# Attention and two MLPs on one core: one transfer per head for q and k, loads reordered, all sum units added on GpSimd

## The chip, the cores and the metric

The kernel runs on one core of a Trainium2 chip. The metric is the device time of one execution in microseconds (us). Five engines work side by side and meet at semaphores: TensorE (PE), VectorE (DVE), ScalarE (ACT), GpSimd (POOL) and SyncE (SP), which here does nothing but issue transfers. Transfers are carried by 16 DMA engines that all queues share.

## The reference

Inputs are q, k and v of 2 batches x 12 heads x 448 rows x 64 in float32, a number `cap` (30), and the weights of two MLPs of 768 and 2048 columns.

```python
scores = np.matmul(q, k.transpose(0, 1, 3, 2)) / np.sqrt(64)
scores = cap * np.tanh(scores / cap)
scores = scores - np.max(scores, axis=-1, keepdims=True)
attn = np.exp(scores)
attn = attn / (np.sum(attn, axis=-1, keepdims=True) + 1e-09)
x = np.matmul(attn, v)            # then heads side by side: 896 x 768
x = relu(x @ w_in1) ** 2 @ w_out1
x = silu(x @ w_in2) @ w_out2
```

## The kernel before

**Work.** The 24 heads are 12 pairs. One "slot" of PE handles one pair: scores of pair j (three pieces of 128 key rows for both heads, one of 64), and, between them, the product of the weights with v of pair j-1 and the sum of its weights. After slot 11 the two MLPs follow, which are matrix products alone: weights are split in a high and a low part (ACT writes `w_hi`, DVE writes `w_lo`), and each product is three matmuls (lines 371 to 373).

**Loading.** A head's rows are dealt to partitions so that partition i holds rows 14i to 14i+13, 896 numbers that lie together in memory. DVE transposes blocks of 32 x 32 (lines 582 and 586 into `qk_f`), and a head dimension of 64 needs two groups of 32 partitions: the first half of every row's 64 columns in one, the second half in the other. The kernel loads the same 32 x 896 numbers twice, into the two groups, the first group shifted by 32 columns, so that one strided view of `qk_raw` reads the first half of the columns in one group and the second in the other. That makes four transfers for k of a pair and four for q (line 190). v takes four transfers of 32 partitions for `v_t` (line 200) and four for `v_x` (line 206). A pair thus takes 16 transfers.

**Order on SP.** k of pair 0, q and k of pair 1, v of pairs 0 and 1, the first two weight tiles (line 212), q and k of pair 2. Then `load_pair(j)` in a loop: wait until pair j-1 is transposed (`s_turned`), load q and k of pair j+1; wait until the sums of pair j-2 are done (`s_att`), load v of pair j. There are two `qk_raw` buffers. q of pair 0 is issued by ACT (line 455).

**Weights and sums.** ACT takes tanh of the scores (lines 464, 467) and the exponential in two pieces (line 472, 1792 and 1344 columns). A pair's weights are 7 units of 448 columns: units 0 to 3 in the first piece, 4 to 6 in the second. POOL adds units 0,1 and 2,3 (line 275) and then, once for each head, the half unit 6 (line 280). PE sums down the partitions with matmuls against ones (`sums`, line 333): two read POOL's sums and two read units 4 and 5 as they are. They leave four groups of 32 partitions, and DVE joins them (`finish`: line 603 copies four pieces into `den_x`, line 605 adds), takes the reciprocal and scales the output.

**What stands late.** ACT's `weight_high` (line 495) for weight tile 0 stands after pair 1, the one for tile 1 between pair 10 and pair 11. PE's first MLP work starts with line 371 after slot 11.

Of the kernel before, what the change touches and what calls it, by code (L numbers as in the profile page):

```python
# [13 lines left out]
P = 128  # L14
DMA = 16


def attention_then_two_mlps(nc, q, k, v, cap, w_in1, w_out1, w_in2, w_out2, out):
# [28 lines left out]

    q_v = q.rearrange("b (m h) (i t) d -> (b m) h i (t d)", h=2, t=QB)
    k_v = k.rearrange("b (m h) (i t) d -> (b m) h i (t d)", h=2, t=QB)
    v_v = v.rearrange("b (m h) (i t) d -> (b m) i h (t d)", h=2, t=QB)  # L50
    w_in_v = [w.rearrange("(k p) f -> p k f", p=P) for w in (w_in1, w_in2)]
# [4 lines left out]
    with ctx:  # L56
# [14 lines left out]
        eps_t = sb(ctx, "eps_t", [P, 1])  # L71
        o_sel = sb(ctx, "o_sel", [P, BL])
        w_raw = [sb(ctx, f"w_raw{i}", [P, WK, P]) for i in range(2)]
# [5 lines left out]
        with ExitStack() as att:  # L79

            qk_raw = [sb(att, f"qk_raw{i}", [P, BL + 2 * QB * D]) for i in range(2)]
# [12 lines left out]
            rowmax = sb(att, "rowmax", [P, 2, S])  # L94
            den_r = sb(att, "den_r", [P, S])
            den_x = sb(att, "den_x", [P, QB])
# [86 lines left out]
        def _(sp):  # L183
            def load_part(j, n, src, done):

                for h in range(2):
                    for a in range(2):
                        at = n * QB * D + BL * (1 - a)
                        rp = slice(D * h + BL * a, D * h + BL * a + BL)
                        sp.dma_start(qk_raw[j.par][rp, at:at + QB * D],  # L190
                                     src[bass.ds(j.no, 1), h][0]).then_inc(done, DMA)

            def load_qk(j):
                load_part(j, 0, k_v, s_qk_in[j.par])
                load_part(j, 1, q_v, s_qk_in[j.par])

            def load_v(j):
                for g in range(C):
                    at = g * CW * D
                    sp.dma_start(v_t[j.par][BL * g:BL * g + BL, :, :],  # L200
                                 v_v[bass.ds(j.no, 1), :, :, at:at + CW * D][0]).then_inc(s_v_in[j.par], DMA)
                for h in range(2):
                    for g in range(XB):
                        at = (MB + g) * D
                        rp = slice(D * h + BL * g, D * h + BL * g + BL)
                        sp.dma_start(v_x[j.par][rp, :],  # L206
                                     v_v[bass.ds(j.no, 1), :, h, at:at + D][0]).then_inc(s_v_in[j.par], DMA)

# [11 lines left out]

            load_part(At(0, 0), 0, k_v, s_first_in[0])
            sp.wait_ge(s_first_in[0], 4 * DMA)
            load_qk(At(0, 1))
            for j in range(2):
                load_v(At(0, j))
            for f in range(2):
                load_w_in(0, At(0, f), At(0, f))
            sp.wait_ge(s_turned, 2)
            load_qk(At(0, 2))

            def load_pair(j):
# [34 lines left out]
        def _(pool):  # L266
# [3 lines left out]
            def add_units(j):  # L270

                wait(pool, s_att, j.no - 1)
                pool.wait_ge(s_exp, 2 * j.no + 1)
                t, a = prob[j.par], asum[j.par]
                pool.tensor_tensor(a[:, :, :], t[:, 0:2, :], t[:, 2:4, :], ALU.add).then_inc(s_sum, 1)
                pool.wait_ge(s_exp, 2 * j.no + 2)
                for h in range(2):
                    rp = slice(D * h, D * h + D)
                    pool.wait_ge(s_sum, 3 * j.no + 1 + h)
                    pool.tensor_tensor(a[rp, h, :], a[rp, h, :], t[rp, 2 * CW, :], ALU.add).then_inc(s_sum, 1)  # L280
                pool.wait_ge(s_sum, 3 * j.no + 3)

# [16 lines left out]
        def _(pe):  # L299
# [27 lines left out]
            def sums(j):  # L327

                pe.wait_ge(s_sum, 3 * j.no + 3)
                for g in range(4):  # L330
                    h = g // 2
                    mov = asum[j.par][:, h, :] if g % 2 == 0 else prob[j.par][:, 4 + h, :]
                    last = pe.matmul(o_t[j.par][BL * g:BL * g + BL, 1, 0:S], o_sel[:, :], mov,  # L333
                                     start=True, stop=True)
                last.then_inc(s_att, 1)

            def output_main(j):
                pe.wait_ge(s_v_in[j.par], 8 * DMA * (j.half + 1))
# [111 lines left out]
        def _(act):  # L450
            for h in range(2):
                for a in range(2):
                    at = QB * D + BL * (1 - a)
                    rp = slice(D * h + BL * a, D * h + BL * a + BL)
                    act.dma_start(qk_raw[0][rp, at:at + QB * D], q_v[0, h]).then_inc(s_first_in[1], DMA)
            off_max = shifted(act)
# [107 lines left out]
        def _(dve):  # L564
            dve.memset(o_sel[:, :], 1.0).then_inc(s_fill, 1)
            dve.memset(eps_t[:, :], EPS).then_inc(s_eps_t, 1)
# [9 lines left out]
            def blocks(j, first, last):  # L576

                return qk_raw[j.par][:, BL + first * D:BL + last * D].rearrange("p (t x) -> p t x", x=D)[:, :, 0:BL]

# [9 lines left out]
            def prepare(j):  # L589
                dve.wait_ge(s_qk_in[j.par], 8 * DMA * (j.half + j.par))  # L590
                wait(dve, s_score, C * (j.no - 1))
# [3 lines left out]
            def finish(j):  # L595

                dve.wait_ge(s_att, j.no + 1)
                dve.transpose(den_r[:, :], o_t[j.par][:, 1, 0:S]).then_inc(s_den, 1)
                dve.wait_ge(s_den, 8 * j.no + 1)
                part = den_r[:, :].rearrange("p (b i) -> p b i", i=BL)[:, :, 0]  # L600
                for g in range(4):
                    o = g + 1 - 2 * (g % 2)
                    dve.tensor_copy(den_x[BL * g:BL * g + BL, :], part[BL * o:BL * o + BL, :]).then_inc(s_den, 1)
                dve.wait_ge(s_den, 8 * j.no + 5)
                dve.scalar_tensor_tensor(den[:, :], part, eps_t[:, 0:1], den_x[:, :],
                                         op0=ALU.add, op1=ALU.add).then_inc(s_den, 1)
                dve.wait_ge(s_den, 8 * j.no + 6)
                dve.reciprocal(den[:, :], den[:, :]).then_inc(s_den, 1)
                dve.wait_ge(s_den, 8 * j.no + 7)
                dve.transpose(rinv[:, :].rearrange("p (b i) -> p b i", i=BL),  # L610
                              den[:, :].unsqueeze(2).to_broadcast([P, QB, BL])).then_inc(s_den, 1)
                dve.wait_ge(s_den, 8 * j.no + 8)
                dve.tensor_tensor(att_o[:, :], o_t[j.par][:, 0, 0:S], rinv[:, :], ALU.mult).then_inc(s_norm, 1)  # L613
# [158 lines left out]
```

## Time and profile before

| | us |
|---|---|
| median of 3 runs | 587.06 (586.62 to 587.24) |
| profiled execution | 586.58 |
| its span in the profile | 584.8 |
| PE busy | 565.7 (97%) |
| DVE / ACT / POOL busy | 223.1 / 167.4 / 54.3 |

The span runs from the first to the last recorded instruction, and 1.8 us of the profiled time lie outside it. In the rows of the timeline a number in front is the start in us, the next the time from the first start to the last end of the merged instructions, and brackets give the idle time just before and what ended it. "SPq" rows are SP's issuing of transfers, not the transfers themselves.

### The profile page before, as it was taken

What the parts mean: (1) busy time and instruction counts of PE and PEld (TensorE: products, weight loads), DVE (VectorE), ACT (ScalarE), POOL (GpSimd) and SP (SyncE); (2) the same over time, 40 slices, a digit from 0 to 9 for tenths busy, and PEclk for the clock granted to TensorE, in tenths of its full rate; (3) what the DMA queues carried; (4) which work ended last, traced back from release to release, by engine and by line L of the source; (5) the groups of instructions that cost most, each with busy time, mean ns of one, the idle gap of its engine ahead of it and who ended that gap; (6) DMA issues with size and microseconds to landing.
All of it is one profiled execution on the core that took longest, in us unless ns stands there. A gap on an engine that the chain in (4) does not pass through costs nothing.

```text
span 584.8 us, 7972 instructions
## 1 busy us (share of the span) xinstructions
PE 565.7 (97%) x2800; PEld 466.0 (80%) x2800; DVE 223.1 (38%) x403; ACT 167.4 (29%) x207; POOL 54.3 (9%) x42
## 2 busy tenths in 40 slices
PE   5599999999999999999999999999999999999996
PEld 3133333499999999999999999999999999999996
DVE  2177977975555555121202123333333302120210
ACT  4578888422222222021202113222222201010100
POOL 1535655400000000000000000000000000000000
PEclk9989999999999999999999999999999999999999
DMA  5745544211111122212121102111112221212553
GB/s 141 188 106 155 146 129 123 67 34 56 54 54 54 55 62 67 69 39 69 41 66 40 49 28 67 56 53 55 54 54 62 62 66 47 62 46 63 92 86 48
DMA packets 83122, 41.93 MB, mean 72 GB/s; under 512 B 27808, under 2 KB 80032, under 8 KB 83104
## 3 DMA queue, kind: packets, MB, share of 16 engines
q1 hardware_dynamic: 81952, 41.13, 26.4%
q10 hardware_dynamic: 1120, 0.57, 0.5%
q8 instruction: 10, 0.16, 0.1%
q14 instruction: 8, 0.07, 0.0%
q0 software_dynamic: 32, 0.00, 0.0%
HBM read 38.93 MB, written 2.75 MB: 71 GB/s over the span
## 4 chain that ended last, share of the span: by engine, by line
PE 90%; SPq 4%; DMA 2%; DVE 2%; issue 1%; DVEq 0%
PE ring L371 13%; PE o_t L371 13%; PE o_t L373 13%; PE ring L373 13%; PE ring L372 13%; PE o_t L372 13%; PE o_t L324 4%; PE ring L312 3%; SPq L190 2%; DMA qk_raw<-in_q_dram 1%; PE o_t L333 1%; PE ring L309 1%; PE o_t L322 1%; SPq L206 1%; DMA qk_raw<-in_k_dram 1%
## 5 line engine op out<-in xcount | busy, mean ns | idle before, releaser
L689 DVE TENSOR_TENSOR w_lo<-w_raw,w_hi 128x768 fp32r<-128x768 f32 (+1 forms) x56 | 60.0, 1072 | 292.6 <-ACT w_hi L495 292.6
L495 ACT ACTIVATE w_hi<-w_raw 128x768 fp32r<-128x768 f32 (+1 forms) x56 | 52.5, 938 | 358.8 <-PE ring L373 182.8
L371 PE MATMUL ring<-x_hi,w_hi 128*128 128x448 f32 x384 | 140.4, 366 | 0.0
L371 PE MATMUL o_t<-g_hi,w_hi 128*128 128x448 f32 x384 | 140.2, 365 | 0.0
L373 PE MATMUL o_t<-g_hi,w_lo 128*128 128x448 f32 x384 | 140.2, 365 | 0.0
L372 PE MATMUL ring<-x_lo,w_hi 128*128 128x448 f32 x384 | 140.2, 365 | 0.0
L372 PE MATMUL o_t<-g_lo,w_hi 128*128 128x448 f32 x384 | 140.2, 365 | 0.0
L373 PE MATMUL ring<-x_hi,w_lo 128*128 128x448 f32 x384 | 140.2, 365 | 0.0
L371 PEld LDWEIGHTS ring<-x_hi,w_hi 128*128 128x128 f32 x384 | 72.1, 188 | 7.2 <-issue 1.5
L372 PEld LDWEIGHTS o_t<-g_lo,w_hi 128*128 128x128 f32 x384 | 72.1, 188 | 5.7
L371 PEld LDWEIGHTS o_t<-g_hi,w_hi 128*128 128x128 f32 x384 | 72.1, 188 | 5.7
L373 PEld LDWEIGHTS o_t<-g_hi,w_lo 128*128 128x128 f32 x384 | 72.1, 188 | 5.7
L373 PEld LDWEIGHTS ring<-x_hi,w_lo 128*128 128x128 f32 x384 | 72.1, 188 | 5.7
L372 PEld LDWEIGHTS ring<-x_lo,w_hi 128*128 128x128 f32 x384 | 72.1, 188 | 5.7
L312 PE MATMUL ring<-qk_f 64*128 64x448 f32 x144 | 35.2, 594 | 11.3 <-DVE qk_f L586 9.1
L467 ACT ACTIVATE prob<-ring,qk_scale 128x896 f32<-128x896 f32 x36 | 35.0, 1002 | 19.5 <-PE ring L312 19.5
L312 PEld LDWEIGHTS ring<-qk_f 64*128 64x128 f32 x144 | 12.6, 193 | 32.9 <-issue 28.4
L472 ACT ACTIVATE prob<-prob,cap_a 128x1792 f32<-128x1792 f32 (+1 forms) x24 | 38.5, 1602 | 0.8
L663 DVE TENSOR_TENSOR g_lo<-work,g_hi 128x448 f32 (+1 forms) x64 | 36.9, 618 | 0.0
L324 PE MATMUL o_t<-prob,v_t 128*64 128x448 f32 x144 | 30.7, 562 | 0.9 <-DVE att_o L613 0.6
L513 ACT ACTIVATE work<-ring 128x448 f32<-128x448 f32 x64 | 30.7, 531 | 0.0
L280 POOL TENSOR_TENSOR asum<-asum,prob 64x448 f32<-64x448 f32 x24 | 28.2, 1177 | 18.3 <-ACT prob L472 17.3
(44 smaller groups left out, 249.9 us busy)
## 6 DMA issues: line engine op xcount, KB each, us to landing
w_raw<-in_moe_w_in_dram SPq DMA_DIRECT2D x32, 384.0 KB, 3.4
w_raw<-in_moe_w_out_dram SPq DMA_DIRECT2D x24, 512.0 KB, 3.9
qk_raw<-in_k_dram SPq DMA_DIRECT2D x48, 112.0 KB, 2.4
qk_raw<-in_q_dram SPq DMA_DIRECT2D x44, 112.0 KB, 2.5
out_dram<-rows SPq DMA_DIRECT2D x46, 56.0 KB, 2.2
v_t<-in_v_dram SPq DMA_DIRECT2D x48, 48.0 KB, 1.8
v_x<-in_v_dram SPq DMA_DIRECT2D x48, 8.0 KB, 1.6
qk_raw<-in_q_dram ACTq DMA_DIRECT2D x4, 112.0 KB, 4.3
```

The costliest lines, as they stand in the source:

```text
L280: pool.tensor_tensor(a[rp, h, :], a[rp, h, :], t[rp, 2 * CW, :], ALU.add).then_inc(s_sum, 1)
L312: last = pe.matmul(ring[2 * (u % 2) + h][:, 0:S], qk_f[j.par][rp, u * P:u * P + P], qk_f[j.par][rp, S:2 * S], start=True, stop=True)
L324: pe.matmul(out_h, v_t[j.par][:, h, c * D:c * D + D], prob[j.par][:, 2 * c + h, :], start=(c == 0), stop=False)
L371: pe.matmul(dst, w_hi[par][:, kk, :], mov_hi, start=start, stop=False)
L372: pe.matmul(dst, w_hi[par][:, kk, :], mov_lo, start=False, stop=False)
L373: return pe.matmul(dst, w_lo[par][:, kk, :], mov_hi, start=False, stop=stop)
L467: act.activation(prob[j.par][:, 2 * u:2 * u + 2, :], ring2[u % 2][:, :, 0:S], ACT.Tanh, scale=qk_scale[:, 0:1]).then_inc(s_ring, 1)
L472: act.activation(t, t, ACT.Exp, scale=cap_a[:, 0:1]).then_inc(s_exp, 1)
L495: act.activation(w_hi[n.par][:, 0:blocks, :], w_raw[n.par][:, 0:blocks, :], ACT.Copy).then_inc(s_w_hi, 1)
L513: act.activation(work[f.par][b][:, :], ring[2 * f.par + b][:, 0:S], ACT.Relu if layer == 0 else ACT.Silu).then_inc(s_ring, 1)
L663: dve.tensor_tensor(g_lo[:, bass.ds(f.no, 1), b, :], work[f.par][b][:, :].unsqueeze(1), g_hi[:, bass.ds(f.no, 1), b, :].bitcast(F32), ALU. ...
L689: dve.tensor_tensor(w_lo[n.par][:, 0:blocks, :], w_raw[n.par][:, 0:blocks, :], w_hi[n.par][:, 0:blocks, :].bitcast(F32), ALU.subtract).the ...
```

## The change

1. **q and k.** One transfer per head fills both groups of 32 partitions. Its source pattern starts with a dimension of count 2 (the two column halves, 32 numbers apart), then 32 rows, then 864 numbers; the destination is 64 partitions x 864. A pair takes four such transfers instead of eight. The bytes are nearly the same (864 instead of 896 numbers a partition), and a transfer carries twice as many.
2. **v.** `v_t` takes one transfer per head: source counts 4, 32, 192, destination 128 partitions. `v_x` takes one per head: source counts 2, 32, 64, destination 64 partitions. A pair takes four instead of eight.
3. **SP's order.** v of pair 1 is issued after q and k of pair 2, and the first two weight tiles after `load_pair(10)` instead of before pair 2. ACT's and DVE's steps for these tiles move with them.
4. **Sums.** POOL adds units 4,5 too, in one more 128 x 896 addition. PE then needs two matmuls of 64 columns for a pair's sums instead of four of 32, and DVE one addition (`eps`) instead of four copies and an addition.

```diff
+    def halves(t):
+        flat = t.rearrange("b (m h) (i t) d -> (b m) h (i t d)", h=2, t=QB)
+        def head(n, h):
+            first = flat[n, h] if isinstance(n, int) else flat[bass.ds(n, 1), h][0]
+            return bass.AP(first.tensor, first.offset, [[BL, 2], [QB * D, BL], [1, QB * D - BL]])
+        return head
+    q_v, k_v = halves(q), halves(k)
+    v_flat = v.rearrange("b (m h) (i t) d -> (b m) h i (t d)", h=2, t=QB)
+    v_main = v_flat[:, :, :, 0:MB * D].rearrange("n h i (g x) -> n h g i x", g=C)
+    v_rest = v_flat[:, :, :, MB * D:QB * D].rearrange("n h i (g x) -> n h g i x", g=XB)
...
             def load_qk(j):
-                load_part(j, 0, k_v, s_qk_in[j.par])
-                load_part(j, 1, q_v, s_qk_in[j.par])
+                for n, src in enumerate((k_v, q_v)):
+                    for h in range(2):
+                        sp.dma_start(qk_raw[j.par][D * h:D * h + D, n * QB * D:(n + 1) * QB * D - BL],
+                                     src(j.no, h)).then_inc(s_qk_in[j.par], DMA)
...
             def load_v(j):
+                for h in range(2):
+                    rp = slice(D * h, D * h + D)
+                    sp.dma_start(v_t[j.par][:, h, :], v_main[bass.ds(j.no, 1), h][0]).then_inc(s_v_in[j.par], DMA)
+                    sp.dma_start(v_x[j.par][rp, :], v_rest[bass.ds(j.no, 1), h][0]).then_inc(s_v_in[j.par], DMA)
...
             load_qk(At(0, 1))
-            for j in range(2):
-                load_v(At(0, j))
-            for f in range(2):
-                load_w_in(0, At(0, f), At(0, f))
+            load_v(At(0, 0))
             sp.wait_ge(s_turned, 2)
             load_qk(At(0, 2))
+            load_v(At(0, 1))
...
             load_pair(At(0, PAIRS - 2))
+            for f in range(2):
+                load_w_in(0, At(0, f), At(0, f))
...
                 pool.wait_ge(s_exp, 2 * j.no + 2)
+                pool.wait_ge(s_sum, 4 * j.no + 1)
+                pool.tensor_tensor(a[:, :, :], a[:, :, :], t[:, 4:6, :], ALU.add).then_inc(s_sum, 1)
...
-                for g in range(4):
-                    h = g // 2
-                    mov = asum[j.par][:, h, :] if g % 2 == 0 else prob[j.par][:, 4 + h, :]
-                    last = pe.matmul(o_t[j.par][BL * g:BL * g + BL, 1, 0:S], o_sel[:, :], mov,
+                for h in range(2):
+                    last = pe.matmul(o_t[j.par][D * h:D * h + D, 1, 0:S], ones[:, :], asum[j.par][:, h, :],
                                      start=True, stop=True)
...
-            weight_high(At(0, 0), KC)
             two_steps(act, 2, PAIRS - 4, weights)
             weights(At(0, PAIRS - 2))
-            weight_high(At(0, 1), KC)
+            for f in range(2):
+                weight_high(At(0, f), KC)
             weights(At(0, PAIRS - 1))
```

SP's queue from its start to the loads of pair 2, before (the shapes are those of the destination; x4 means four in a row; `s_first_in` is the arrival of k of pair 0, `s_turned` the transposes of pair 0):

```order
L190 DMA qk_raw<-in_k_dram 32x896 x4
L190 DMA qk_raw<-in_k_dram 32x896 [waits s_first_in0]
L190 DMA qk_raw<-in_k_dram 32x896 x3
L190 DMA qk_raw<-in_q_dram 32x896 x4
L200 DMA v_t<-in_v_dram 32x2x192 x4
L206 DMA v_x<-in_v_dram 32x64 x4
L200 DMA v_t<-in_v_dram 32x2x192 x4
L206 DMA v_x<-in_v_dram 32x64 x4
L212 DMA w_raw<-in_moe_w_in_dram 128x6x128 x2
L190 DMA qk_raw<-in_k_dram 32x896 [waits s_turned]
L190 DMA qk_raw<-in_k_dram 32x896 x3
L190 DMA qk_raw<-in_q_dram 32x896 x4
```

The same place now:

```order
L218 DMA qk_raw<-in_k_dram 64x1x864 x2
L196 DMA qk_raw<-in_k_dram 64x1x864 [waits s_first_in0]
L196 DMA qk_raw<-in_k_dram 64x1x864
L196 DMA qk_raw<-in_q_dram 64x1x864 x2
L202 DMA v_t<-in_v_dram 128x1x192
L203 DMA v_x<-in_v_dram 64x1x64
L202 DMA v_t<-in_v_dram 128x1x192
L203 DMA v_x<-in_v_dram 64x1x64
L196 DMA qk_raw<-in_k_dram 64x1x864 [waits s_turned]
L196 DMA qk_raw<-in_k_dram 64x1x864
L196 DMA qk_raw<-in_q_dram 64x1x864 x2
```

Between the arrival of k of pair 0 and the first load of pair 2 stood 26 transfers, and now there are 8.

ACT's queue from the end of pair 10 to the start of pair 11, before (`s_w_in1` is the arrival of weight tile 1, `s_score` a finished piece of scores):

```order
L472 ACTIVATE prob<-prob,cap_a 128x1344 [waits s_ring]
L484 UNCONDITIONAL_BRANCH
L495 ACTIVATE w_hi<-w_raw 128x768 [waits s_w_in1]
L467 ACTIVATE prob<-ring,qk_scale 128x896 [waits s_att,s_score]
L467 ACTIVATE prob<-ring,qk_scale 128x896 [waits s_score]
```

The same place now:

```order
L466 ACTIVATE prob<-prob,cap_a 128x1344 [waits s_ring]
L478 UNCONDITIONAL_BRANCH
L489 ACTIVATE w_hi<-w_raw 128x768 [waits s_w_in0]
L489 ACTIVATE w_hi<-w_raw 128x768 [waits s_w_in1]
L461 ACTIVATE prob<-ring,qk_scale 128x896 [waits s_att,s_score]
L461 ACTIVATE prob<-ring,qk_scale 128x896 [waits s_score]
```

The step for tile 0 stood after pair 1 and is now here too, so both wait ahead of pair 11's first tanh.

## Rows read from the trace of the kernel before

**Rows 1.** The page, busy shares and 40 slices of 14.6 us

```profile
PE 565.7 (97%) x2800; PEld 466.0 (80%) x2800; DVE 223.1 (38%) x403; ACT 167.4 (29%) x207; POOL 54.3 (9%) x42
...
PE   5599999999999999999999999999999999999996
...
PEclk9989999999999999999999999999999999999999
DMA  5745544211111122212121102111112221212553
```

**Rows 2.** Timeline of PE: starts of slots 1, 2, 3, 4, 5, 11, then the MLP

```profile
14.31 1.77 PE L312 MATMUL ring<-qk_f 64*128 64x448 f32 x8 [0.88 <-ACT prob L467]
...
28.68 3.36 PE L312 MATMUL ring<-qk_f 64*128 64x448 f32 x8 [6.70 <-DVE qk_f L586]
...
38.82 1.77 PE L312 MATMUL ring<-qk_f 64*128 64x448 f32 x8
...
46.42 1.77 PE L312 MATMUL ring<-qk_f 64*128 64x448 f32 x8
...
54.02 1.77 PE L312 MATMUL ring<-qk_f 64*128 64x448 f32 x8
...
100.72 1.77 PE L312 MATMUL ring<-qk_f 64*128 64x448 f32 x8
...
108.58 0.47 PE L371 MATMUL ring<-x_hi,w_hi 128*128 128x448 f32 x1
```

**Rows 3.** Timeline of DVE, the transposes of pair 2

```profile
27.37 0.58 DVE L582 STREAM_TRANSPOSE qk_f<-qk_raw 128x384 f32<-128x384 f32 x1 [13.27 <-DMA qk_raw<-in_q_dram]
27.87 0.67 DVE L586 STREAM_TRANSPOSE qk_f<-qk_raw 128x512 f32<-128x512 f32 x1
```

**Rows 4.** Timeline of SP's queue

```profile
0.75 8.05 SPq L190 DMA_DIRECT2D qk_raw<-in_k_dram  x8
8.84 1.81 SPq L190 DMA_DIRECT2D qk_raw<-in_q_dram  x4
...
21.20 1.81 SPq L190 DMA_DIRECT2D qk_raw<-in_q_dram  x4
```

**Rows 5.** The page, issues of transfers: count, KB each, us to landing

```profile
w_raw<-in_moe_w_in_dram SPq DMA_DIRECT2D x32, 384.0 KB, 3.4
...
qk_raw<-in_q_dram SPq DMA_DIRECT2D x44, 112.0 KB, 2.5
...
v_x<-in_v_dram SPq DMA_DIRECT2D x48, 8.0 KB, 1.6
```

**Rows 6.** Two stretches: busy us, PEclk, DMA share of 16 engines, GB/s

```profile
22.00:27.00 5.00, 0.00 (x0) 0.00 (x0) 0.00 (x0) 1.35 (x2) 2.25 (x2) 1.00 1.07 241
40.00:100.00 60.00, 59.28 (x312) 18.65 (x312) 48.63 (x93) 51.74 (x48) 35.06 (x24) 1.00 0.48 138
```

**Rows 7.** Transfers in 34.0 to 34.4 us: rate, then share of 16 engines

```profile
DMA packets 35, 0.08 MB, mean 188 GB/s; under 512 B 14, under 2 KB 14, under 8 KB 35
...
q1 hardware_dynamic: 35, 0.08, 51.9%
```

**Rows 8.** Timelines of ACT, POOL and PE round one pair's sums

```profile
53.17 1.42 ACT L472 ACTIVATE prob<-prob,cap_a 128x1344 f32<-128x1344 f32 x1
...
54.75 2.38 POOL L280 TENSOR_TENSOR asum<-asum,prob 64x448 f32<-64x448 f32 x2 [1.30 <-ACT prob L472]
58.90 2.07 POOL L275 TENSOR_TENSOR asum<-prob 128x896 f32<-128x896 f32 x1 [1.77 <-ACT prob L472]
...
60.82 0.56 PE L333 MATMUL o_t<-asum,o_sel 128*32 128x448 f32 x1
```

**Rows 9.** Timeline of ACT before slot 11's tanh

```profile
101.19 0.83 ACT L495 ACTIVATE w_hi<-w_raw 128x768 fp32r<-128x768 f32 x1
101.92 1.88 ACT L467 ACTIVATE prob<-ring,qk_scale 128x896 f32<-128x896 f32 x2
```

More of the change, by code:

```diff
@@ L45, in attention_then_two_mlps @@
     assert PAIRS % 2 == 0 and FC % 2 == 0 and KC == 6
-    q_v = q.rearrange("b (m h) (i t) d -> (b m) h i (t d)", h=2, t=QB)
-    k_v = k.rearrange("b (m h) (i t) d -> (b m) h i (t d)", h=2, t=QB)
-    v_v = v.rearrange("b (m h) (i t) d -> (b m) i h (t d)", h=2, t=QB)
+    def halves(t):
[8 more added lines that the diff above has]
+    v_rest = v_flat[:, :, :, MB * D:QB * D].rearrange("n h i (g x) -> n h g i x", g=XB)
     w_in_v = [w.rearrange("(k p) f -> p k f", p=P) for w in (w_in1, w_in2)]
@@ L71, in attention_then_two_mlps @@
         eps_t = sb(ctx, "eps_t", [P, 1])
-        o_sel = sb(ctx, "o_sel", [P, BL])
+        ones = sb(ctx, "ones", [P, D])
         w_raw = [sb(ctx, f"w_raw{i}", [P, WK, P]) for i in range(2)]
@@ L79, in attention_then_two_mlps @@
         with ExitStack() as att:
-            qk_raw = [sb(att, f"qk_raw{i}", [P, BL + 2 * QB * D]) for i in range(2)]
+            qk_raw = [sb(att, f"qk_raw{i}", [P, 2 * QB * D]) for i in range(2)]
             v_t = [sb(att, f"v_t{i}", [P, 2, CW * D]) for i in range(2)]
@@ L95, in attention_then_two_mlps @@
             den_r = sb(att, "den_r", [P, S])
-            den_x = sb(att, "den_x", [P, QB])
             den = sb(att, "den", [P, QB])
@@ L183, in _, with load_qk, load_v @@
         def _(sp):
-            def load_part(j, n, src, done):
-                for h in range(2):
[L187 to L193, printed above, removed]
-                load_part(j, 0, k_v, s_qk_in[j.par])
-                load_part(j, 1, q_v, s_qk_in[j.par])
[L197 to L207, printed above, removed]
+            def load_qk(j):
+                for n, src in enumerate((k_v, q_v)):
+                    for h in range(2):
+                        sp.dma_start(qk_raw[j.par][D * h:D * h + D, n * QB * D:(n + 1) * QB * D - BL],
+                                     src(j.no, h)).then_inc(s_qk_in[j.par], DMA)
+            def load_v(j):
+                for h in range(2):
+                    rp = slice(D * h, D * h + D)
+                    sp.dma_start(v_t[j.par][:, h, :], v_main[bass.ds(j.no, 1), h][0]).then_inc(s_v_in[j.par], DMA)
+                    sp.dma_start(v_x[j.par][rp, :], v_rest[bass.ds(j.no, 1), h][0]).then_inc(s_v_in[j.par], DMA)
             def load_w_in(layer, f, n):
@@ L219, in load_w_out @@
                              ).then_inc(s_w_in[n.par], DMA)
-            load_part(At(0, 0), 0, k_v, s_first_in[0])
-            sp.wait_ge(s_first_in[0], 4 * DMA)
+            for h in range(2):
+                sp.dma_start(qk_raw[0][D * h:D * h + D, 0:QB * D - BL], k_v(0, h)).then_inc(s_first_in[0], DMA)
+            sp.wait_ge(s_first_in[0], 2 * DMA)
             load_qk(At(0, 1))
-            for j in range(2):
-                load_v(At(0, j))
-            for f in range(2):
-                load_w_in(0, At(0, f), At(0, f))
+            load_v(At(0, 0))
             sp.wait_ge(s_turned, 2)
             load_qk(At(0, 2))
+            load_v(At(0, 1))
             def load_pair(j):
@@ L276, in add_units @@
                 pool.wait_ge(s_exp, 2 * j.no + 2)
+                pool.wait_ge(s_sum, 4 * j.no + 1)
+                pool.tensor_tensor(a[:, :, :], a[:, :, :], t[:, 4:6, :], ALU.add).then_inc(s_sum, 1)
                 for h in range(2):
                     rp = slice(D * h, D * h + D)
-                    pool.wait_ge(s_sum, 3 * j.no + 1 + h)
+                    pool.wait_ge(s_sum, 4 * j.no + 2 + h)
                     pool.tensor_tensor(a[rp, h, :], a[rp, h, :], t[rp, 2 * CW, :], ALU.add).then_inc(s_sum, 1)
-                pool.wait_ge(s_sum, 3 * j.no + 3)
+                pool.wait_ge(s_sum, 4 * j.no + 4)
             with pool.If(shifted(pool)):
@@ L327, in sums @@
             def sums(j):
-                pe.wait_ge(s_sum, 3 * j.no + 3)
-                for g in range(4):
-                    h = g // 2
-                    mov = asum[j.par][:, h, :] if g % 2 == 0 else prob[j.par][:, 4 + h, :]
-                    last = pe.matmul(o_t[j.par][BL * g:BL * g + BL, 1, 0:S], o_sel[:, :], mov,
+                pe.wait_ge(s_sum, 4 * j.no + 4)
+                for h in range(2):
+                    last = pe.matmul(o_t[j.par][D * h:D * h + D, 1, 0:S], ones[:, :], asum[j.par][:, h, :],
                                      start=True, stop=True)
@@ L337, in output_main @@
             def output_main(j):
-                pe.wait_ge(s_v_in[j.par], 8 * DMA * (j.half + 1))
+                pe.wait_ge(s_v_in[j.par], 4 * DMA * (j.half + 1))
                 wait(pe, s_norm, j.no - 1)
@@ L451, in _ @@
             for h in range(2):
[L452 to L455, printed above, removed]
+                act.dma_start(qk_raw[0][D * h:D * h + D, QB * D:2 * QB * D - BL], q_v(0, h)).then_inc(s_first_in[1], DMA)
             off_max = shifted(act)
@@ L564, in _ @@
         def _(dve):
-            dve.memset(o_sel[:, :], 1.0).then_inc(s_fill, 1)
+            dve.memset(ones[:, :], 1.0).then_inc(s_fill, 1)
             dve.memset(eps_t[:, :], EPS).then_inc(s_eps_t, 1)
@@ L576, in blocks @@
             def blocks(j, first, last):
-                return qk_raw[j.par][:, BL + first * D:BL + last * D].rearrange("p (t x) -> p t x", x=D)[:, :, 0:BL]
+                return qk_raw[j.par][:, first * D:last * D].rearrange("p (t x) -> p t x", x=D)[:, :, 0:BL]
             def turn_main(j):
@@ L589, in prepare @@
             def prepare(j):
-                dve.wait_ge(s_qk_in[j.par], 8 * DMA * (j.half + j.par))
+                dve.wait_ge(s_qk_in[j.par], 4 * DMA * (j.half + j.par))
                 wait(dve, s_score, C * (j.no - 1))
@@ L598, in finish @@
                 dve.transpose(den_r[:, :], o_t[j.par][:, 1, 0:S]).then_inc(s_den, 1)
[L599 to L607, printed above, removed]
+                dve.wait_ge(s_den, 4 * j.no + 1)
+                dve.tensor_scalar(den[:, :], den_r[:, :].rearrange("p (b i) -> p b i", i=BL)[:, :, 0],
+                                  eps_t[:, 0:1], None, ALU.add).then_inc(s_den, 1)
+                dve.wait_ge(s_den, 4 * j.no + 2)
                 dve.reciprocal(den[:, :], den[:, :]).then_inc(s_den, 1)
-                dve.wait_ge(s_den, 8 * j.no + 7)
+                dve.wait_ge(s_den, 4 * j.no + 3)
                 dve.transpose(rinv[:, :].rearrange("p (b i) -> p b i", i=BL),
                               den[:, :].unsqueeze(2).to_broadcast([P, QB, BL])).then_inc(s_den, 1)
-                dve.wait_ge(s_den, 8 * j.no + 8)
+                dve.wait_ge(s_den, 4 * j.no + 4)
                 dve.tensor_tensor(att_o[:, :], o_t[j.par][:, 0, 0:S], rinv[:, :], ALU.mult).then_inc(s_norm, 1)
@@ L690, in weight_low @@
                                   w_hi[n.par][:, 0:blocks, :].bitcast(F32), ALU.subtract).then_inc(s_w_lo, 1)
-            dve.wait_ge(s_first_in[0], 4 * DMA)
+            dve.wait_ge(s_first_in[0], 2 * DMA)
             turn_main(At(0, 0)).then_inc(s_turned, 1)
-            dve.wait_ge(s_first_in[1], 4 * DMA)
+            dve.wait_ge(s_first_in[1], 2 * DMA)
             turn_rest(At(0, 0), MB, 2 * QB).then_inc(s_turned, 1)
@@ L708, in _ @@
             shift(At(0, 1))
-            weight_low(At(0, 0), KC)
             two_steps(dve, 2, PAIRS - 4, slot)
@@ L712, in _ @@
             shift(At(0, PAIRS - 1))
+            weight_low(At(0, 0), KC)
+            finish(At(0, PAIRS - 3))
             weight_low(At(0, 1), KC)
-            for j in range(PAIRS - 3, PAIRS):
+            for j in range(PAIRS - 2, PAIRS):
                 finish(At(0, j))
```

## The prediction, made before the result was known

> **What bounds the kernel now.** I read the page first [rows 1]: PE is busy 97% of the span, and its slices show 9 from the third on. Only the first slices are open, and there PE waits. So a gain can only come from the time before the MLPs, and a loss too. Then the timeline of PE [rows 2]: slot 2 starts at 28.68 after 6.70 us of idle time, slots 3 and 4 follow 7.60 us apart, slot 11 starts at 100.72 and the MLP at 108.58. From there on PE works through to the end, whatever happened before. The end therefore moves by as much as the start of slot 11 moves, plus what slot 11 itself loses.
>
> What slot 2 waits for is in DVE's timeline [rows 3]: its transposes had waited 13.27 us for the arrival of q. SP's queue tells why [rows 4]: a transfer costs SP 0.45 us (1.81 for four), and 26 of them stand between the arrival of k of pair 0 and the first load of pair 2. In the steady slots no row shows PE waiting for data, and the DMA engines are half busy: share 0.48 at 138 GB/s [rows 6].
>
> **Transfers of q and k.** This is the term that decides. Today each starts, on both sides, with a count of 32. Its 112 KB land 2.5 us after the issue, where 8 KB land after 1.6 [rows 5]; if one or two engines carried the 112 KB, at the rates below, they would add 2.3 us or more instead of 0.9. So they are spread widely. The new transfers start at the source with a count of 2 (`v_t`: 4, `v_x`: 2). If the hardware deals out a transfer over its engines by that leading count, two engines carry all of q and k, and the other 14 stand by. No row shows a transfer that leads with so small a count. I hold this for likely, because the leading counts are the only thing in which these patterns differ in kind from all that the trace shows spread.
>
> The Trainium skill speaks against this change here: DMA: Bandwidth & Descriptors, section "Why a DMA increments its semaphore by 16 and not by 1", says that a transfer uses the largest number of engines up to 16 that divides the slowest count (other than 1) of both sides, and that they are the lowest-numbered ones. By it q, k and `v_x` would run on two engines and `v_t` on four, all sharing the same two; that no row here shows such a case leaves it open.
>
> The price, from rows. Bytes for one of the two engines: q and k of a pair are 4 transfers x 64 partitions x 3456 B = 885 KB, half of it 442 KB. v is 2 x 98 KB over four engines and 2 x 16 KB over two, 65.5 KB for one engine. Before slot 11 can start, q and k of 12 pairs and v of pairs 0 to 9 have to pass (SP's order puts v of pair 10 behind q and k of pair 11): 12 x 442 + 10 x 65.5 = 5963 KB. The rate of one busy engine is the GB/s divided by 16 x share: 241 / 17.1 = 14.1 where all are full, 138 / 7.7 = 18.0 in the steady slots [rows 6], and 188 / 8.3 = 22.6 in a short stretch at half load [rows 7]. The rate rises as fewer are active, so for two of sixteen I take 25, somewhat over the best row. That is 5963 / 25 = 238.5 us. Bounds: 14.1 gives 423, 18.0 gives 331. On the fast side no row excludes more than 25, and I allow a quarter more, 31: 192 us. The same page of the Trainium skill, section "Specifications", has about 27 GiB/s for one engine; by that the same bytes would take 206 us, and the sum would come out near 702.
>
> Around it: 0.75 to the first issue and 1.6 of fixed time [rows 4, 5], 2.4 us; one gap after pair 0, since SP waits for k of pair 0 before it issues pair 1, 0.5 + 1.6 = 2.1 us; two transposes at the end, 0.58 + 0.67 = 1.3 [rows 3]. Slot 11 starts at 2.4 + 238.5 + 2.1 + 1.3 = 244.3 instead of 100.72 [rows 2], 143.6 later. Later loads leave no gap: q and k of pair j+1 are issued when pair j-1 is transposed, while those of pair j (18 us of work) still stand in the queue.
>
> **PE after long waits.** Slot 2, which follows 6.70 us of idle time, took 38.82 - 28.68 = 10.14 us where the next took 7.60: the eight first matmuls ran 3.36 instead of 1.77 us [rows 2], and the clock row has an 8 there [rows 1]. In the new kernel PE waits some 10 us before each slot, and only slot 11's loss counts: 10.14 - 7.60 = 2.5 us.
>
> **Weights loaded late.** The steps of ACT for both weight tiles now stand before pair 11's first tanh, and wait for arrival. Behind q and k of pair 11 stand v of pair 10 (65.5 KB for one engine) and two tiles of 384 KB, spread over 16 (24.6 KB each): 115 / 25 = 4.6 us, 1.6 fixed, and two steps of 0.83 [rows 9], 7.9 us after arrival. The tanh would else start about 2.9 after it (transposes 1.3, first scores at the low clock 1.6); but PE's next need for it, the third scores, comes only after the products with v, some 6.5 us after arrival, against 7.9 + 0.9 for the first tanh now. The rest is 2.3 us. If the tiles arrive earlier, it is nothing.
>
> **Sums and DVE.** POOL gets another 2.08 us per pair [rows 8]. Its end moves from 57.1 to 59.2-odd, and PE wants it at 60.82: it is hidden, with 1.5 us left; and the next pair's first addition would start at 59.3 instead of 58.90, while the one after waits for ACT anyhow. PE's sums drop from four to two matmuls that run side by side; 0 to 0.1 us a slot, and where PE waits for data, nothing. DVE loses five small instructions off the path. SP issues 8 transfers fewer per pair, about 3.6 us, which no longer matters when the engines are the bound.
>
> **Sum.** 143.6 + 2.5 + 2.3 = 148.4. On the profiled 586.58 (its span 584.8) that is 735.0, and the median of the runs shown is 587.06, 0.5 above it. I predict 735.
>
> **Rivals.**
>
> *A. The transfers are spread as before (faster).* Then the reordering pays: between k of pair 0 and the loads of pair 2 SP has 8 transfers instead of 26, so pair 2 arrives some 10 us earlier, and slot 2 starts when slot 1 ends. That returns 6.70 us of idle time and the 2.5 us of low clock, and sums give up to 1.1 more over 11 slots (I take 0.6): 586.6 - 9.8 = 576.8. For it: bytes are the same, and the rows show nothing against it. Against it: the leading count, above. Chance 0.13.
>
> *B. Two engines, and they idle between pairs.* If a queue holds only so much of the long transfers, SP stands still in issuing, and each pair's loads begin only after the last ones have been transposed: 0.5 + 1.6 + 1.25 = 3.35 us for each of 10 pairs, 33.5 us on top: 768. For it: 64 rows x 4 now lie on one engine's queue. Against it: two buffers and the order of SP's waits. Chance 0.08.
>
> *C. Spread, but POOL becomes the bound.* If POOL keeps its 1.30 us wait for ACT between its additions, a pair takes 2.08 + 1.30 + 2.08 + 2.38 = 7.8 us, just over the slot; at 1 us a slot for 9 slots the gain of A is eaten: about 586. For it: POOL's time per pair goes up by half. Against it: the slack of 1.5 us [rows 8]. Chance 0.02.
>
> *Forecast.* Two engines, always busy: 735. Chance 0.77.
>
> **How the numbers follow.** The forecast's own range goes from 31 GB/s an engine (689) to 18.0 (828), and rivals B lies inside. I give 690 to 835. Outside lie A and C (0.15) and a slower engine (0.05). About 0.2% is what a measurement of this kernel can tell from no change. Faster by more is A, 0.13; within is C, 0.02; slower is the rest, 0.85.
>
> **What would show it.** In the profile after, DMA share in the attention slices should fall to about 2/16 = 0.12 with some 50 GB/s, and PE, DVE and ACT should be idle more than half of the time there, DVE's transposes waiting for q or k by some 10 us a pair; slot 11 should start near 244 us; landings of q and k should be 15 us or more; the MLP's time from its first matmul to the end should stay at 584.8 - 108.6 = 476. If the landings stay near 2.5 us and slot 2 starts near 22 us, A holds. If the share is low, but shows gaps between pairs, B holds. If q and k land after some 10 us and the start of slot 11 lies near 200, the mechanism is right and the engine's rate was set too low.

## The result and the profile after

| | before | changed |
|---|---|---|
| median of the runs, us | 586.98 (586.62 to 587.24) | 731.52 (731.14 to 732.12) |
| profiled execution / its span, us | 586.58 / 584.8 | 731.61 / 729.8 |
| start of slot 11, us from the span's start | 100.72 | 241.22 |
| first matmul of the MLPs, us from the span's start | 108.58 | 251.69 |

The ratio is 1.2464, with a 95% interval of 1.2442 to 1.2486. The forecast was 735. One execution of all those below, 599.4 us of the kernel with a leading count of 8, is a slow one and left out of its figures.

The page of the changed kernel, to set beside [rows 1]: the engines' busy time, then 40 slices, now of 18.2 us each.

```profile
PE 593.3 (81%) x2752; PEld 473.9 (65%) x2752; DVE 200.4 (27%) x355; ACT 169.1 (23%) x207; POOL 78.5 (11%) x54
...
PE   2355544444455799999999999999999999999997
...
PEclk9997767777777799999999999999999999999999
DMA  1111111111111302121222111112121222121253
GB/s 43 52 55 55 56 53 56 56 56 56 57 57 56 113 22 65 43 65 43 79 57 58 57 55 37 45 44 65 44 65 43 65 57 58 57 58 58 71 83 56
```

In the first 13 slices PE is busy for two to five tenths of the time, and the DMA engines carry some 55 GB/s at a share of 0.1-odd, slice after slice. The one slice with a 3 and 113 GB/s is the one in which the first weight tiles, spread over all engines, are loaded. Nothing looks busy, and that is how two full engines among idle ones look in a mean over 16 (that it is two is shown below).

The starts of slots in PE's timeline, as in [rows 2], and the first matmul of the MLPs:

```profile
41.35 3.36 PE L311 MATMUL ring<-qk_f 64*128 64x448 f32 x8 [10.86 <-DVE qk_f L580]
...
221.37 3.36 PE L311 MATMUL ring<-qk_f 64*128 64x448 f32 x8 [9.91 <-DVE qk_f L580]
241.22 3.36 PE L311 MATMUL ring<-qk_f 64*128 64x448 f32 x8 [9.63 <-DVE qk_f L580]
251.69 0.47 PE L368 MATMUL ring<-x_hi,w_hi 128*128 128x448 f32 x1
```

The last two slots lie 19.85 us apart where [rows 2] have 7.60, and each starts after some 10 us of waiting for DVE's transposes, with the eight first matmuls at 3.36 instead of 1.77 us (the granted clock is 0.74 in the mean of the stretch below, where [rows 6] have 1.00). DVE in turn waited for q; the same line as in [rows 3]:

```profile
200.26 0.58 DVE L576 STREAM_TRANSPOSE qk_f<-qk_raw 128x384 f32<-128x384 f32 x1 [15.06 <-DMA qk_raw<-in_q_dram]
220.14 0.58 DVE L576 STREAM_TRANSPOSE qk_f<-qk_raw 128x384 f32<-128x384 f32 x1 [15.01 <-DMA qk_raw<-in_q_dram]
239.99 0.58 DVE L576 STREAM_TRANSPOSE qk_f<-qk_raw 128x384 f32<-128x384 f32 x1 [14.98 <-DMA qk_raw<-in_q_dram]
```

100 us of steady slots, to set beside [rows 6] (busy us of PE, PEld, DVE, ACT, POOL, then PEclk, DMA share, GB/s):

```profile
100.00:200.00 100.00, 48.80 (x180) 15.52 (x180) 22.34 (x45) 33.75 (x30) 31.92 (x20) 0.74 0.15 56
```

56 GB/s at a share of 0.15 is 23 GB/s for a busy engine. The other way of reckoning goes by the bytes: if two engines carry q and k, each of them gets 508 KB a pair (442 of q and k, 65.5 of v), and 508 KB every 19.99 us (41.35 to 241.22, ten slots) is 25.4 KB a us.

The page's chain of waits names another culprit:

```profile
PE 66%; SPq 27%; DMA 5%; issue 1%; DVE 0%
SPq L203 12%; PE ring L368 11%; PE ring L370 11%; PE ring L369 11%; PE o_t L370 11%; PE o_t L369 11%; PE o_t L368 11%; SPq L196 8%; SPq L202 6%; DMA qk_raw<-in_q_dram 3%; DMA qk_raw<-in_k_dram 2%; PE o_t L323 1%; PE ring L311 1%; PE o_t L330 0%; PE o_t L321 0%
```

27% of the span are put down to SP's issuing, and SP's timeline has single issues of 3.8 to 4.9 us:

```profile
141.39 2.72 SPq L196 DMA_DIRECT2D qk_raw<-in_q_dram  x2
144.38 3.83 SPq L202 DMA_DIRECT2D v_t<-in_v_dram  x1
148.40 3.90 SPq L203 DMA_DIRECT2D v_x<-in_v_dram  x1
152.50 0.57 SPq L202 DMA_DIRECT2D v_t<-in_v_dram  x1
153.26 4.86 SPq L203 DMA_DIRECT2D v_x<-in_v_dram  x1
```

That gives two readings. Theory 1: the leading count deals q and k to two engines, these are full, and SP stands because their queues are full. Theory 2: long transfers of 64 partitions are slow in themselves, or SP's stalls are the cause. These views can't part them.

### The profile page after: what moved, and what is told of

Read it like the earlier page. It is cut to its first block, busy times and chain, and to the rows that moved or that the text cites. A ratio compares the mean times of both kernels' runs of the same rounds, so it can differ in the third digit from the quotient of the medians.

```text
span 729.8 us, 7646 instructions
## 1 busy us (share of the span) xinstructions
PE 593.3 (81%) x2752; PEld 473.9 (65%) x2752; DVE 200.4 (27%) x355; ACT 169.1 (23%) x207; POOL 78.5 (11%) x54
## 4 chain that ended last, share of the span: by engine, by line
PE 66%; SPq 27%; DMA 5%; issue 1%; DVE 0%
SPq L203 12%; PE ring L368 11%; PE ring L370 11%; PE ring L369 11%; PE o_t L370 11%; PE o_t L369 11%; PE o_t L368 11%; SPq L196 8%; SPq L202 6%; DMA qk_raw<-in_q_dram 3%; DMA qk_raw<-in_k_dram 2%; PE o_t L323 1%; PE ring L311 1%; PE o_t L330 0%; PE o_t L321 0%
## 5 line engine op out<-in xcount | busy, mean ns | idle before, releaser
L311 PE MATMUL ring<-qk_f 64*128 64x448 f32 x144 | 53.3, 866 | 129.4 <-DVE qk_f L580 128.3
L370 PE MATMUL ring<-x_hi,w_lo 128*128 128x448 f32 x384 | 140.5, 366 | 0.0
L369 PE MATMUL ring<-x_lo,w_hi 128*128 128x448 f32 x384 | 140.5, 366 | 0.0
L311 PEld LDWEIGHTS ring<-qk_f 64*128 64x128 f32 x144 | 18.2, 278 | 157.5 <-issue 120.9
L576 DVE STREAM_TRANSPOSE qk_f<-qk_raw 128x384 f32<-128x384 f32 x12 | 6.9, 578 | 187.7 <-DMA qk_raw<-in_q_dram 176.2
L272 POOL TENSOR_TENSOR asum<-prob 128x896 f32<-128x896 f32 x12 | 25.3, 2107 | 152.5 <-ACT prob L466 152.5
L323 PE MATMUL o_t<-prob,v_t 128*64 128x448 f32 x144 | 37.4, 664 | 0.0
```

What stands on the lines that cost most here:

```text
L311: last = pe.matmul(ring[2 * (u % 2) + h][:, 0:S], qk_f[j.par][rp, u * P:u * P + P], qk_f[j.par][rp, S:2 * S], start=True, stop=True)
L323: pe.matmul(out_h, v_t[j.par][:, h, c * D:c * D + D], prob[j.par][:, 2 * c + h, :], start=(c == 0), stop=False)
L369: pe.matmul(dst, w_hi[par][:, kk, :], mov_lo, start=False, stop=False)
L370: return pe.matmul(dst, w_lo[par][:, kk, :], mov_hi, start=False, stop=stop)
```

## Experiments

Every kernel was timed together with the kernel before, whose median was 586.4 in all three series. The expectations were written before the runs. Where they say that the MLPs take 466.2 or 468.5 us, that is a time over the last 2304 matmuls of PE, which takes in a few of the attention and leaves out as many of the MLPs; from the start of the first to the start of the last matmul of their own lines the MLPs take 471.2 us in the kernel before and 472.8 in the changed one, and these are the numbers used below.

### The leading count, alone

```diff
-            return bass.AP(first.tensor, first.offset, [[BL, 2], [QB * D, BL], [1, QB * D - BL]])
+            return bass.AP(first.tensor, first.offset, [[16, 4], [QB * D * 2, 16], [1, QB * D - BL]])
```

**A count of 4.** 

> The changed kernel with one edit: the source pattern of q and k leads with a count of 4 instead of 2 (4 x 16 rows x 864 instead of 2 x 32 x 864). Number of transfers, bytes, destination and every wait stay; other rows of the head are read than should be, so the output is not the reference's. Theory 1 (the leading count sets how many engines carry a transfer): q and k run on 4 engines, an engine has 12 x 221 + 10 x 65.5 = 3307 KB before slot 11 instead of 5963, 2656 KB less, at the 25.5 KB a us that one engine did here (508 KB every 19.95 us) 104 us less: 627, and a pair every 11.2 us. Theory 2 (long transfers of 64 partitions are slow in themselves, or SP's stalls in issuing them are the bound): nothing changes, 731.

**A count of 8** (`[[8, 8], [QB * D * 4, 8], ...]`). 

> The changed kernel with a leading count of 8 for q and k (8 x 8 rows x 864; other rows than should be are read, so the output is not the reference's). Theory 1: an engine has 110.6 + 65.5 = 176 KB a pair, 6.9 us at 25.5 KB a us, less than a slot's 7.6, so the engines are no longer the bound: 579 to 583, near the leading count of 16 (579.1), where the count of 4 gave 634.8. If the time went by the count in proportion instead: about 605.

**A count of 16** (`[[4, 16], [QB * D * 8, 4], ...]`). 

> As the last, with a leading count of 16 (16 x 4 rows x 864; the output is not the reference's). Theory 1: q and k run on all 16 engines, v stays on four and two (65.5 KB or 2.6 us of one engine per pair, hidden); the reordering pays at last and the time falls below the kernel before, to 577. Theory 2: 731, as in the changed kernel, since transfers, sizes and issues are the same.

These three kernels read other rows of a head than they should, so they show the time alone.

| leading count of q, k | time, us | ratio to before (95%) | one slot, us | KB a pair for the engine with most |
|---|---|---|---|---|
| 2 (the change) | 731.5 | 1.246 (1.244 to 1.249) | 19.99 | 508 |
| 4 | 634.8 | 1.082 (1.080 to 1.083) | 11.8 | 287 |
| 8 | 590.2 | 1.007 (1.004 to 1.010) | 8.05 | 176 |
| 16 | 579.1 | 0.987 (0.986 to 0.989) | 7.62 | 121 |

(Slots: means from slot 1 to slot 11 with a count of 2, from slot 2 to slot 11 with the others.) Theory 2 asked for 731 in each. Number, size and destination of the transfers are the same in all four, so it falls. Only the cut of the source pattern differs, and it moves the time by 152 us.

The cut also changes which rows are read, so the times alone leave room for a rival: that the other addresses are the faster ones. The traces settle this. Each keeps the events by which q's and k's semaphores were raised, though no view prints them:

| kernel | transfers of q and k of pairs 1 to 11 | events | events for one transfer |
|---|---|---|---|
| before | 88 | 1408 | 16 |
| changed, count 2 | 44 | 132 | 3 |
| count 4 | 44 | 220 | 5 |
| count 8 | 44 | 396 | 9 |
| count 16 | 44 | 704 | 16 |

In the changed kernel one of the three events comes with SP's issue, and two come later, 0.4 to 1.4 us apart. For the four transfers of pair 5 the early ones stand at 101.06, 101.89, 102.52 and 104.69, and the others at 106.97 and 107.67, 111.19 and 111.98, 115.42 and 116.18, 119.69 and 120.41. Read as one event for each engine that carries a part, that is 2, 4, 8 and 16 engines for the four counts, so Theory 1 stands. The new transfers of v, with 192 events for 48 transfers in all, fit four engines for `v_t` and two for `v_x` (24 x 5 + 24 x 3).

The stretches, with counts of 4, 8 and 16 in this order:

```profile
20.00:140.00 120.00, 87.07 (x350) 27.71 (x352) 44.08 (x77) 68.75 (x62) 65.55 (x41) 0.88 0.26 96
```

```profile
40.00:90.00 50.00, 48.26 (x230) 15.37 (x227) 42.27 (x59) 40.96 (x38) 42.44 (x26) 1.00 0.42 144
```

```profile
20.00:95.00 75.00, 75.00 (x356) 23.86 (x354) 56.85 (x83) 65.89 (x61) 65.80 (x40) 1.00 0.56 147
```

The rate goes from 56 to 96 GB/s with the count doubled; 0.26 of 16 engines are 4. The count of 4 came out 7.8 us over the expected 627: 287 KB every 11.8 us is 24.3 KB a us, not 25.5. The count of 16 came out 2.1 over the expected 577. With 8 the fullest engines need 6.9 us of a slot's 7.6 by estimate (176 KB at 25.5 KB a us), so they are off the bound in the mean, but PE still waits 0.2 to 1.0 us here and there for `v_x` or for DVE, and nine executions spread from 586.6 to 594.8, where 16 gives 578.9 to 579.6. The expected 579 to 583 for 8 was wrong. In the profiled executions its MLPs start 8.8 us later than with 16, 4.7 of them gone before slot 2 starts (27.12 against 22.39), and the rest lost in slots 2 to 11.

SP's issues in the kernel with a count of 16, by the same lines of code as above:

```profile
42.39 1.18 SPq L196 DMA_DIRECT2D qk_raw<-in_q_dram  x2
45.35 0.58 SPq L202 DMA_DIRECT2D v_t<-in_v_dram  x1
46.12 0.57 SPq L203 DMA_DIRECT2D v_x<-in_v_dram  x1
46.80 0.56 SPq L202 DMA_DIRECT2D v_t<-in_v_dram  x1
47.55 0.55 SPq L203 DMA_DIRECT2D v_x<-in_v_dram  x1
```

The issues of 3.8 to 4.9 us are gone though these instructions are the same. SP's stall was a consequence of full engines, and the chain had put the engines' work down to the one that waited for room.

### As many transfers as before, still leading with 2

```diff
+                        for c in range(2):
+                            at = n * QB * D + c * ((QB * D - BL) // 2)
+                            sp.dma_start(qk_raw[j.par][D * h:D * h + D, at:at + (QB * D - BL) // 2],
+                                         src(j.no, h, c)).then_inc(s_qk_in[j.par], DMA)
```

> The changed kernel with each transfer of q and k cut in two by columns (2 x 32 rows x 432 numbers, eight transfers a pair as before the change, 108 KB each, all still leading with a count of 2). Theory 1: the same two engines carry the same bytes, 731; a little more, up to 760, if rows of 1728 B cost an engine more per byte than rows of 3456 B. Theory 2 (length and number of the transfers are the cause): with as many transfers of the same size as before the change, most of the loss goes, under 620.

739.39 us, a ratio of 1.2603 (1.2585 to 1.2622). Eight transfers of 108 KB a pair are as bad as four of 216 KB; slots lie 20.7 us apart, so twice as many transfers with rows of half the length cost 0.7 us a pair more. Length and number are not the cause of the loss.

### The old transfers with the rest of the change

Lines 189 to 205 of this kernel are those of the kernel before; SP's order, the late weights and the new sums stay.

> The changed kernel with the transfers of q, k and v of the kernel before (16 a pair, each leading with 32), keeping SP's new order, the late weights and all sums on GpSimd. Theory 1: all of the loss goes, slot 2 follows slot 1 without a wait: 577, as rival A of the prediction has it, perhaps 1.5 us more, because the MLPs took 1.6 us longer in the changed kernel than before. Theory 3 (the sums on GpSimd or the order carry part of the loss): over 587.

589.42 us (587.49 to 591.22), ratio 1.0054 (1.0037 to 1.0071). Of the loss of 145 us 142 are gone, but the gain of rival A isn't there either: the expected 577 was missed, and Theory 3 (over 587) holds. Where the gain went was the next question.

### Order and sums, each alone

> The kernel before with SP's new order and the weight tiles loaded late, transfers and sums as before. The run with all old transfers (old_transfers) did not gain the 9 us of the start: its slots lay 8.0 us apart, ACT stood 3.2 us before slot 11's last scores, and its MLPs took 2.3 us longer from the first matmul to the last (468.5 against 466.2). Theory P (SP's queue bounds the slots: 16 issues of 0.45 us and its waits): slot 2 starts at 22 to 24, slots stay 8.0 apart, 583. Theory S (the GpSimd sums, which make DVE late and PE wait for att_o, cost it): slots 7.6 apart, 577. Either way the MLPs take 466.2 if their 2.3 us belong to the sums' edit.

587.18 us, ratio 1.0005 (0.9996 to 1.0015): no difference, and neither the 583 of Theory P nor the 577 of Theory S. PE's timeline, slots 2, 3, 10 and 11, and the MLPs:

```profile
23.19 1.77 PE L312 MATMUL ring<-qk_f 64*128 64x448 f32 x8
30.79 1.77 PE L312 MATMUL ring<-qk_f 64*128 64x448 f32 x8
...
89.27 1.77 PE L312 MATMUL ring<-qk_f 64*128 64x448 f32 x8
97.37 1.77 PE L312 MATMUL ring<-qk_f 64*128 64x448 f32 x8
109.18 0.47 PE L371 MATMUL ring<-x_hi,w_hi 128*128 128x448 f32 x1
```

The start is gained: slot 3 begins at 30.79 instead of 38.82 [rows 2], 8.0 us earlier. Then it is given back twice. Slots 3 to 11 lie 8.3 us apart on average, against 7.7 before (4.7 us in all), while SP issues with short pauses only:

```profile
56.60 1.74 SPq L190 DMA_DIRECT2D qk_raw<-in_k_dram  x4
58.43 1.76 SPq L190 DMA_DIRECT2D qk_raw<-in_q_dram  x4
60.44 1.84 SPq L200 DMA_DIRECT2D v_t<-in_v_dram  x4
62.50 1.95 SPq L206 DMA_DIRECT2D v_x<-in_v_dram  x4
64.72 1.74 SPq L190 DMA_DIRECT2D qk_raw<-in_k_dram  x4
```

And slot 11 takes 11.8 us instead of 7.9, because ACT waits for the late weight tiles and PE for ACT:

```profile
99.79 0.84 ACT L495 ACTIVATE w_hi<-w_raw 128x768 fp32r<-128x768 f32 x1 [1.87 <-DMA w_raw<-in_moe_w_in_dram]
101.36 0.84 ACT L495 ACTIVATE w_hi<-w_raw 128x768 fp32r<-128x768 f32 x1 [0.72 <-DMA w_raw<-in_moe_w_in_dram]
...
104.04 1.42 PE L312 MATMUL ring<-qk_f 64*128 64x448 f32 x4 [2.40 <-ACT prob L467]
```

8.0 - 4.7 - 3.9 is -0.6 us, which is what the start of the MLPs shows (109.18 against 108.58). The 3.9 us are a place where an early start met transfers that could not keep up, and the 4.7 us may be another. SP's loads of k for pairs 3 to 11 begin 8.31 us apart on average here (22.42 to 88.89), as the slots do, each 7.8 to 9.0 us ahead of its slot. In the kernel before SP is hardly faster (8.12 us a pair for pairs 5 to 11, 43.56 to 92.30), but it is further ahead: by 10.5 us for pair 5, of which 8.4 are left for pair 11. With 12 issues a pair instead of 16 slots lie 7.8 to 7.9 us apart, and with 8 and a count of 16 they lie 7.62 apart. So it is likely that SP's issuing sets the pace. It is not shown: in these slots PE's own waits name DVE's `att_o`.

The sums alone: 

> The kernel before with the new sums alone (all units on GpSimd, two matmuls of 64 columns, five fewer small instructions on DVE, ones of 64 columns instead of 32). If the longer MLP belongs to this edit: 468.5 us from its first matmul to its last, and 588.7 in all. If also the slots suffer (GpSimd 6.5 us busy of each 7.7): 590 to 592. If it is hidden, as the prediction said: 586 to 587.

589.09 us, ratio 1.0045 (1.0030 to 1.0059). The slots are 7.6 to 8.0 us up to slot 10 and 8.15 for slot 11, and the MLPs start at 108.57, as before; the time is in the MLPs, whose instructions the edit doesn't touch.

### Where a tile lies

```diff
-        o_sel = sb(ctx, "o_sel", [P, BL])
+        o_sel = sb(ctx, "o_sel", [P, D])
...
+                    last = pe.matmul(o_t[j.par][BL * g:BL * g + BL, 1, 0:S], o_sel[:, 0:BL], mov,
```

> The kernel before with one edit: the tile of ones is declared 64 wide instead of 32 and still used 32 wide, so that all tiles allocated behind it (weights, work tiles, the hidden layer) lie 128 B further in each partition. No instruction changes its work. Theory L (the 2.3 us by which the MLPs are longer in all five kernels with the new sums come from where the tiles lie): MLPs 468.5 us from the first matmul to the last, 588.7 in all. Theory W (they come from the work): 466.2, and 586.5.

588.42 us, ratio 1.0031 (1.0020 to 1.0042), with MLPs of 472.8 us.

The other way round, the new sums with the old places:

```diff
-        ones = sb(ctx, "ones", [P, D])
+        pad = sb(ctx, "pad", [P, BL])
...
+            ones = sb(att, "ones", [P, D])
```

> The kernel before with the new sums alone, as sums_only (589.1), but the wide tile of ones lies among the attention's tiles and a tile of 32 columns keeps its old place, so that weights, work tiles and hidden layer lie where they did. Theory L: MLPs 466.2, 586.8 in all. Theory W: 468.5 and 589.

586.73 us, ratio 1.0004 (0.9994 to 1.0013), with MLPs of 471.2 us. In the same 100 us of the first MLP layer the kernel with the wide tile does 492 matmuls and the one with the old places 495 (PE busy and count come second):

```profile
130.00:230.00 100.00, 100.00 (x492) 92.05 (x492) 50.86 (x97) 22.48 (x39) 0.00 (x0) 1.00 0.20 59
```

```profile
130.00:230.00 100.00, 100.00 (x495) 92.69 (x494) 50.51 (x96) 22.95 (x40) 0.00 (x0) 1.00 0.20 59
```

So 1.55 us come from 128 B of place, and Theory L holds in its kind: the size is 1.55 us and not the 2.3 that the expectations name, which was read off the last 2304 matmuls. The sums themselves cost nothing and gain nothing that can be told from noise, with GpSimd's 2.1 us more a pair.

### Fewer issues for v

> The kernel before with the new transfers for v alone (four a pair on four and two engines; order, q, k and sums as before). SP has 8 transfers fewer in front of pair 2 (3.6 us) and four fewer in each slot. If SP's queue bounds the start and the slots: slot 2 starts at 25 instead of 28.7, slots 7.6 to 7.7 apart, 582 to 584. If v on few engines costs as much as it saves: 586.

587.98 us, ratio 1.0022 (1.0012 to 1.0032): slightly slower than before. Slot 2 starts at 29.43, not at 25. One reading is that the expectation forgot to add up v: at the start v of two pairs puts 131 KB on the two engines that q and k of pair 2 need as well, 5 us at 25 KB a us, more than SP's 3.6 us saved. Another is that SP was not what bound the start: in the kernel before all engines are full while pair 2 is loaded (a share of 1.07 [rows 6]). Neither was tried apart.

> The changed kernel with the old transfers for q and k (eight a pair, leading with 32, 16 engines) and the new ones for v (four a pair, on four and two engines), new order and new sums. SP issues 12 transfers a pair, about 5.6 us, so it no longer bounds the slots: slots 7.6 apart. Theory P: 579, as with the leading count of 16. If v on few engines costs time: over 585. If the sums cost it (theory S): 587 to 589.

584.23 us, ratio 0.9957 (0.9943 to 0.9972): a gain of 2.2 us, not down to 579. Slot 2 starts at 26.97; PE had waited 3.24 us for `v_x` in slot 1. In its slots PE waits for `att_o` three times, 0.4 to 0.6 us each.

> The kernel before with the new order and the new transfers for v (12 transfers a pair), old q and k, old sums. Theory P: slots 7.6 to 7.7 apart, slot 2 at 22 to 23, MLPs 466.2 long: 577, about 2 us less than the last one. Theory S: the same. If few engines for v cost time: over 582.

582.41 us (581.96 to 582.93), ratio 0.9929 (0.9912 to 0.9945): 0.7% less than before and clear of noise, though 5 us short of the expected 577. It keeps q and k on 16 engines, takes 12 issues a pair, and leaves sums and places as they were; its MLPs start at 104.01 and take 471.2 us. Slots 3 to 11 lie 7.8 us apart, and ACT's wait for the weight tiles shrinks to 0.28 and 0.39 us.

## Why the prediction was right

**The mechanism.** It rested on one thing that no row showed, that a transfer is dealt out by its leading count. The series of 2, 4, 8 and 16 shows it, and so do the 3, 5, 9 and 16 events for one transfer. The share of 0.15 and 56 GB/s (0.12 and 50 were named), slot 11 near 244 (241.22) and the waits of PE of some 10 us came as forecast. The landing times named as a sign, 15 us or more, stand on no page, but the events give them: for pair 5 the first transfer of q, issued from 101.58, was complete at 116.18, 14.6 us later, and the first of k, issued from 98.92, at 107.67, 8.7 us later. The sign was about right for q and too high for k. Rival B (engines idle between pairs) is out, since an engine moved 25.4 KB a us in the mean over ten slots and 26 KB a us while q and k passed (110.6 KB between landings 4.2 to 4.3 us apart), which leaves no gap of 3.35 us; its condition, SP standing in its issues, was there all the same, without price. Rival A was right on the start, and wrong in its price: 9.8 us, of which `order_only` returned none and the kernel with a count of 16, which has half the issues, 7.4. Rival C's own sum doesn't come out: 7.8 us against a slot of 7.6 is 0.2 a slot and 2 us over nine slots, not 1 and 9. Its condition didn't come up either: `sums_same_places`, with GpSimd's longer sums, took 586.73 us.

**The sum, term by term** (us):

| term | forecast | measured |
|---|---|---|
| slot 11 later by | 143.6 | 140.5 |
| low clock in slot 11, and late weights | 2.5 + 2.3 | 2.6 together |
| MLPs and their end | 0 | 1.9 |
| sum | 148.4 | 145.0 |

The 25 KB a us, set above every row of before, was 25.4: 5963 KB take 3.7 us less at that rate, against the 3.1 us by which the first term came out lower. The rows gave the direction, 14.1 with all engines full and 18.0 and 22.6 at half load [rows 6, 7]; the last step to 25 was an allowance without a row, and that it came within 2% was partly luck. The average of the steady slots, 18.0, would have missed by 96 us. That the total lies only 3.5 us off owes something to luck too, since the first two terms were too high by 5.3 us together and the third too low by 1.9. By an estimate from the some 27 GiB/s of the Trainium skill (DMA: Bandwidth & Descriptors, section "Specifications") the time would have been 702 us; the measured 25.4 KB a us lies 12% below it, for rows of 3456 B with v's shorter rows among them.

**Late weights** cost less than 2.3 us. ACT took its first tanh of pair 11 at 246.19, 6.2 us after arrival, instead of 8:

```profile
244.27 0.84 ACT L489 ACTIVATE w_hi<-w_raw 128x768 fp32r<-128x768 f32 x1 [12.20 <-DMA w_raw<-in_moe_w_in_dram]
...
245.44 0.84 ACT L489 ACTIVATE w_hi<-w_raw 128x768 fp32r<-128x768 f32 x1 [0.32 <-DMA w_raw<-in_moe_w_in_dram]
...
246.19 1.89 ACT L461 ACTIVATE prob<-ring,qk_scale 128x896 f32<-128x896 f32 x2
```

PE's third scores of slot 11 came 7.0 us after its start, where slot 2 of before, with as low a clock, needed 6.7: 0.3 us. The term was real in another kernel: in `order_only`, with the old transfers and the new order, slot 11 took 3.9 us more.

**The step that was missing** is the position of the tiles: 1.55 us of the last term (the other 0.3 lie behind the last matmul and were not looked into). It is 1% of this change, but for an edit worth one or two us it could turn the sign.

## What to carry to other kernels

Before merging transfers, look at the first count of the source pattern (other counts on the destination's side were not tried): merged transfers that lead with 2 ran on two engines of sixteen here, and the kernel with them took 142 us more than with the old transfers, though they move nearly the same bytes with half the issues. In this profile a low DMA share with a flat low rate, and a reader that always waits, meant a few full engines; the chain named the issuing queue, whose stall was a symptom. And when a start-up stall is removed, ask at once which queue runs out next: here 8.0 us were gained at the start and 8.6 given back.

## What the runs showed that was not expected

- A tile declared 32 columns wider, with no change in any instruction's work, made the MLPs 1.55 us longer (471.2 to 472.8 us), all of it in the two layers that read `x_hi` and `x_lo`: 492 instead of 495 matmuls in 100 us of the first. Everything behind it lay 128 B further. Which of the tiles matters was not tried.
- An issue costs SP 0.45 us for the old patterns, 0.53 to 0.66 us for the new ones, with a count of 16 too (1.31 for two of k), and 3.8 to 5.2 us at times when the engines it goes to are full.
- Eight engines that need 90% of a slot's time by estimate were not enough: 590.2 us with a spread of 8.2 us between executions, against 579.1 with a spread of 0.6 on sixteen. How much of it is the start and how much the slots' reserve was not tried apart.
